# Attention and two feed-forward layers on one core: unread products among the lead's small steps, and window loads four slots later

## The chip, the cores and the metric

One core of one Trainium2 chip. The time is device microseconds of that core, for one launch that computes everything. The core has TensorE (matrix products into PSUM), VectorE, ScalarE and GpSimd, and SyncE (SP), whose queue issues all of this kernel's DMAs in program order.

## What is computed

Inputs q, k, v are 4 batches x 8 heads x 576 positions x 64, in f32.

```python
q_d, k_d, v_d = (a.reshape(B, H, Sd, 4, D).mean(axis=3) for a in (q, k, v))
out_up = np.repeat(sm_attn(q_d, k_d, v_d), 4, axis=2)      # coarse attention
mask = np.abs(pos[:, None] - pos[None, :]) < 4             # local attention
out_local = softmax(where(mask, scale * q @ k.T, -1e9)) @ v
x = (out_up + out_local) as (B, S, 512)
x = x + relu(layernorm(x) * g_ln @ w_ch1) @ w_ch2          # first layer, 512 -> 2048 -> 512
x_prev = x shifted by one position
k2 = relu((mu_k * x + (1 - mu_k) * x_prev) @ w_k)          # second layer, 512 -> 1024 -> 512
out = sigmoid((mu_r * x + (1 - mu_r) * x_prev) @ w_r) * ((k2 * k2) @ w_v)
```

## The kernel before

The 2304 rows are worked on in eight units u of 288 rows (half a batch each); a unit has three windows of 96 rows, 24 windows in all. In the layers each f32 operand is split into a high and a low part, and every product is three fast ones (`prods`, L1062): high by high, high by low, low by high.

**The lead.** Unit 0's attention comes first, written out by hand on each engine. On TensorE (from L1160) it is: transposes of k and q (`turn`), local scores (`scores`), coarse scores (`scores_d`), transposes of the probabilities (`turn_p` for local, `turn_d` for coarse ones), the added values of half the heads (`add_values`), the value products (`values`, `values_d`), and at the end three products with ones that sum x over its features (`mean_first`). Between them the other engines mask, exponentiate, sum and copy. `FIRST` (L66) lists these steps with the pair of PSUM banks each uses: 0 is psA, 1 is psH, 2 and 3 are the halves of psY. The small steps use the first bank of their pair, except where `[:, 1]` or both are named; `added_bank` is the second bank of pair 2 until ScalarE has copied it (`added_o`, which signals `vd_first`). `masked` counts VectorE's masked scores.

**The first layer** has 128 steps m (unit u = m // 16, f = m % 16): `up_b(m)` makes 128 hidden features in psH by 12 products, `down_b(m - 1)` adds the features before to psY by 12 more. Between these two halves `attend(slot)` does small pieces of the next unit's attention: slot 2m and 2m + 1, 32 slots for a unit. `LATER` (L74) lists the slot of each piece: for unit u, relative to slot 32(u - 1), scores at 5 and 11, turns at 13 and 19, coarse values at 15, value products AV(u,0) at 15 and AV(u,1) at 21 (windows 1 and 2 of the unit together), the mean at 24. Unit 1's pieces come two slots later (`BEHIND`). `variance(0)` of unit 0 comes in slot 2, behind `up_b(1)`; it needs the sum of squares `sq_sum(0)` that GpSimd makes.

**What feeds the pieces.** All in the order of the slots too:

- `load_later(j)` (L588): a raw quarter of q or k in eight DMAs into one of three buffers `raw`. It waits until VectorE has transposed (`flip`, L1486) the piece three places before. `FLIPS` gives the slots, relative to slot 32u, so before the slot in which the layer takes up unit u: k at -18, -16, -14, -12 for even units alone, q at -10 and -7 for all; `FLIPS_THIRD` is unit 2's, k at -12, -10, -8, -4 and q at -3, -1. So k pieces for units 2, 4, 6 are loaded in the slots in which units 1, 3, 5 are attended.
- `load_v_sum(b, g)` (L600): values for the coarse attention, one DMA into `v_raw`, once GpSimd has summed (`v_sum`) the one before. `V_LOAD` and `V_SUM` give the slots.
- `load_window(w)` (L608): the local values of window w in four DMAs into `v_win`, which has two buffers from window 3 on. It waits for the value product that last read the buffer (`av_done`), so AV(u,0) is followed by the load of window 3u + 2, which AV(u,1) reads, and AV(u,1) by those of windows 3u + 3 and 3u + 4. `values` waits for each window that it reads (`wait_vw`).

SP's program (from L688) goes through the slots and issues in each, in this order, the raw pieces, the sums' values, the windows, and the small loads and stores of the layer. It waits in program order, so what stands behind a wait waits too.

**The second layer** follows with tiles of 512 rows; the change doesn't touch it.

Of the kernel before, what the change touches and what calls it, by code (L numbers as in the profile page):

```python
# [21 lines left out]
def fused_kernel(nc, q, k, v, g_ln, w_ch1, w_ch2, mu_k, mu_r, w_k, w_v, w_r, od_scr, x2_scr, out):  # L22
# [14 lines left out]
    NW_U = 3  # L37
# [52 lines left out]
    ROOT_OUT, ROOT_IN = 3, 10  # L90
    BEHIND = 2

    TURN = {"Tk": [(0, 1), (2, 3), (4, 5)], "Tq": [(0,), (1, 2)]}

    later = []
# [32 lines left out]
    def flips_at(slot):  # L128
        return [x[1:] for x in flips_by_slot if x[0] == slot]
# [8 lines left out]
    def steps_at(slot):  # L138
        return [x[1:] for x in later if x[0] == slot]
# [25 lines left out]
    V_SUM, V_LOAD = {}, {}  # L165
    for b in range(1, B):
        behind = BEHIND if b == 1 else 0
        for g, (s, load) in enumerate(((16 + behind, 8), (22 + behind, 17 + behind), (28 + behind, 21 + 2 * behind), (39, 31))):
            V_SUM[SLOTS * (2 * b - 2) + s] = (b, g)
            V_LOAD[SLOTS * (2 * b - 2) + load] = (b, g)  # L170

# [19 lines left out]
    with ExitStack() as ctx:  # L191
        def sem(name):
            return ctx.enter_context(nc.semaphore(name))

        def sb(scope, name, shape, dt=F32):
            return scope.enter_context(nc.sbuf_tensor(name, shape, dt))
# [60 lines left out]
        kT = sb(ctx, "kT", [P, KT, S])  # L257
# [9 lines left out]
        ident = sb(ctx, "ident", [P, P])  # L267
# [20 lines left out]
        pairs = [psA[:], psH[:], psY[:, 0:2], psY[:, 2:4]]  # L288
# [33 lines left out]
        vd_first = sem("vd_first")  # L322
# [12 lines left out]
        masked = sem("masked")  # L335
# [157 lines left out]
        def turn_source(what, n, x):  # L493
            return (k_first if what == "Tk" else q_first)[0:W, TURN[what][n][x]]

# [85 lines left out]
        def _(sp):  # L581
            def load_first(what, n, x):
                t0 = TURN[what][n][x] * W
                src = (k if what == "Tk" else q)[0, :, t0:t0 + W, :]
# [103 lines left out]
            for slot in range(-LEAD, SLOTS * NU):  # L688
                for x_ in flips_at(slot):
                    if HALF <= flip_of[x_] < len(flips) - RAW:  # L690
                        load_later(flip_of[x_] + RAW)
                if slot in V_LOAD:
                    load_v_sum(*V_LOAD[slot])
                for kind, u, n in steps_at(slot):
                    for part in parts_of(kind, u, n):
                        if kind == "AV" and NW_U * u + part + 2 < NWIN:
                            load_window(NW_U * u + part + 2)
                for kind, u, _ in steps_at(slot - ROOT_OUT):
                    if kind == "V":
                        store_rstd(u)  # L700
                if slot >= SLOTS and slot % SLOTS == 1:
                    store_x2(slot // SLOTS - 1)
                for kind, u, _ in steps_at(slot - ROOT_IN):
                    if kind == "V":
                        load_rstd(u)
                if slot == SLOTS * (NU - 1) + 2:
                    sp.wait_ge(av_done, count_by("AV", NU))
                    sp.wait_ge(x_made, NWIN)
                    sp.wait_ge(lead_zero, 1)
                    load_shifted(0)  # L710
                    load_shifted(1)
                f = slot - SLOTS * (NU - 1)
                if f in (8, 16):
                    j = f // 8 - 1
                    sp.wait_ge(h_ready, M_LAST + 4 * (j + 1))
                    sp.dma_start(wk_raw[:, :, j * 512:(j + 1) * 512],
                                 w_k[:, j * 512:(j + 1) * 512].rearrange("(a p) f -> p a f", p=P)).then_inc(wk_in[j], 16)
                    sp.wait_ge(h_used, M_LAST + 4 * (j + 1))
                    sp.dma_start(wv_raw[:, 4 * j:4 * j + 4],
                                 w_v[512 * j:512 * (j + 1), :].rearrange("(a p) e -> p a e", p=P)).then_inc(wv_in[j], 16)  # L720
                if f == 24:
                    sp.wait_ge(h_ready, M_LAST + 12)
                    sp.dma_start(wr_raw[:, :, :], w_r.rearrange("(a p) f -> p a f", p=P)).then_inc(wr_in, 16)
            store_x2(NU - 1)

            for c in range(NC):
                g0, n = tiles[c]
# [160 lines left out]
        def _(pe):  # L888
            mm = nc.tensor.matmul

            def turn(what, n):
                i = place_of[what, 0, n]
                pe.wait_ge(first_in[turn_of[what, 0, n]], 16 * len(TURN[what][n]))
                wait_bank_out(pe, i)
                for x in range(len(TURN[what][n])):
                    src = turn_source(what, n, x)
# [21 lines left out]
            def turn_d(u, n):  # L918
                i = place_of["PdT", u, n]
                pe.wait_ge(d_normed, 2 * u + n + 1)  # L920
                wait_bank_out(pe, i)
                p = coarse(prob_slot("Sd", u, n), u, n)
                for par in range(2):
                    for j in range(2):
                        for kh in range(2):
                            at = (2 * j + kh) * GU
                            ins = nc.tensor.transpose(pairs[pair_at(i)][0:GU, par, at:at + GU], p[:, par, j, kh * GU:(kh + 1) * GU],  # L927
                                                      ident[0:GU, 0:GU])
                ins.then_inc(pdt_done, 1)

            def add_values():
                for half in range(2):
# [49 lines left out]
            def turn_p(u, n):  # L982
                i = place_of["PT", u, n]
                w = NW_U * u + n
                pe.wait_ge(normed, w + 1)
                wait_bank_out(pe, i)
                p = prob_slot("S", u, n)[0:ROWS]
                for j in range(KT):
                    ins = nc.tensor.transpose(turned_bank(i)[:, j * ROWS:(j + 1) * ROWS],  # L989
                                              p[:, 2 * j * RB:2 * j * RB + RB + KB], ident[0:ROWS, 0:ROWS])  # L990
                ins.then_inc(pt_done, 1)

            def values(u, n):
                i = place_of["AV", u, n]
                for part in parts_of("AV", u, n):
                    pe.wait_ge(pt_out, NW_U * u + part + 1)
                    wait_vw(pe, NW_U * u + part)
                wait_bank_out(pe, i)
                for part in parts_of("AV", u, n):
                    vw = vw_slot(NW_U * u + part)  # L1000
                    pt = turned_place("PT", u, part)
                    place = local_place("AV", u, part, BQ)
                    for j in range(KT):
                        for par in range(2):
                            for bl in range(BLOCKS):
                                row = RB * (par ^ bl)
                                keys = slice(row, row + KB)
                                at = j * ROWS + bl * RB
                                ins = mm(place[D * par:D * par + D, bl, j], vw[keys, bl, j, :], pt[keys, at:at + BQ],  # L1009
                                         start=True, stop=True, skip_group_check=True)  # L1010
                ins.then_inc(av_done, 1)
# [5 lines left out]
            def mean_first(n):  # L1017
                i = place_of["M", 0, n]
                if n + 1 < NW_U:
                    pe.wait_ge(x_summed, n + 1)  # L1020
                else:
                    pe.wait_ge(last_summed, 1)
                wait_bank_out(pe, i)
                mm(pairs[pair_at(i)][:, 0, 0:W], ones[:], xs[:, 0, n * W:(n + 1) * W], start=True, stop=True).then_inc(mean_done, 1)
# [146 lines left out]
            turn_p(0, 0)  # L1171
            add_values()
            turn_d(0, 0)
            turn_d(0, 1)
            values(0, 0)
            turn_p(0, 1)
            values_d(0, 0)
            values_d(0, 1)
            turn_p(0, 2)
            values(0, 1)  # L1180
            values(0, 2)
            pe.wait_ge(consts, 7)
            mean_first(0)
            mean_first(1)
            mean_first(2)
            for slot in range(-LEAD, 0):
                attend(slot)
            for m in range(M_ALL):
# [21 lines left out]
        def _(act):  # L1210
            copy = nc.scalar.copy

            def turn_o(what, n):
                i = place_of[what, 0, n]
                act.wait_ge(turned, turn_of[what, 0, n] + 1)
                c0, nx = TURN[what][n][0], len(TURN[what][n])
                src = pairs[pair_at(i)][:, 0:nx, 0:KT * W].rearrange("p x (j y) -> p x j y", y=W)
# [251 lines left out]
        def _(dve):  # L1469
# [11 lines left out]
            def sum_first(what, n):  # L1481
                dve.wait_ge(turn_out, turn_of[what, 0, n] + 1)
                src, dst = (kT, kdT) if what == "Tk" else (qT, qdT)
                group_sum(src, dst, TURN[what][n][0] * GW, len(TURN[what][n]) * GW)

# [342 lines left out]
```

## Time and profile before

| | us |
|---|---|
| median of 3 runs (lowest to highest) | 768.27 (767.16 to 768.62) |
| the profiled execution | 768.22 |
| its span, first to last instruction | 766.0 |
| TensorE busy | 751.8 |
| VectorE, ScalarE, GpSimd busy | 431.0, 272.6, 232.3 |

The profile is one execution. A group of instructions is named by its line, its engine (PE is TensorE, DVE VectorE, ACT ScalarE, POOL GpSimd, SPq SP's queue) and out<-in by the kernel's names. Matrix products are pipelined: their records overlap, and a product's own duration is longer than the distance to the next. The granted clock of TensorE is given as a share of 2.4 GHz.

### The profile page before, as it was taken

To read this page: it belongs to the slowest core of one execution; us is meant where nothing else is said; L and a number is where in the kernel's file an instruction comes from. 1 tells how busy PE (TensorE), PEld (TensorE's weight loads), DVE (VectorE), ACT (ScalarE), POOL (GpSimd) and SP (SyncE) were. 2 spreads that over 40 slices of the span, in tenths; PEclk is the share of its full clock that TensorE was granted. 3 is DMA by queue.
4 is the path that set the end of the run, shared out by engine and by line. 5 is a ranking of instruction groups with operands and counts; after the bars stand their busy time and mean duration, and the time that the engine had idled before them with its cause. 6 is when DMAs were issued, how large, how long until landed. Compare 5 with 4: busy or idle time off the path is not lost.

```text
span 766.0 us, 15806 instructions
## 1 busy us (share of the span) xinstructions
PE 751.8 (98%) x6433; PEld 693.8 (91%) x6433; DVE 431.0 (56%) x805; ACT 272.6 (36%) x620; POOL 232.3 (30%) x268
## 2 busy tenths in 40 slices
PE   7799999999999999999999999999999999999998
PEld 6699999999999999999999999998888888888886
DVE  5676764444654354554354332567686676766655
ACT  3665423223233223233233231546334434333322
POOL 5666753132444223345223222004111111111101
PEclk9699999999999999999999999999999999999999
DMA  9992451220440121341011003612003011010010
GB/s 188 236 288 59 80 116 18 47 60 11 89 109 20 29 41 55 65 99 40 14 26 39 15 2 138 231 56 87 0 1 110 0 52 33 0 56 1 0 56 28
DMA packets 116543, 49.67 MB, mean 65 GB/s; under 512 B 95084, under 2 KB 105592, under 8 KB 116472
## 3 DMA queue, kind: packets, MB, share of 16 engines
q1 hardware_dynamic: 116472, 48.68, 24.8%
q8 instruction: 51, 0.84, 0.5%
q14 instruction: 20, 0.16, 0.1%
HBM read 39.20 MB, written 9.45 MB: 64 GB/s over the span
## 4 chain that ended last, share of the span: by engine, by line
PE 93%; SPq 2%; DVE 2%; DMA 1%; POOL 1%; issue 1%; ACT 0%; DVEq 0%; ACTq 0%
PE psH L1081 26%; PE psY L1098 25%; PE psH L1132 13%; PE psY L1153 13%; PE psA L1114 6%; PE psA L978 2%; PE psA L1009 2%; PE psA L954 1%; PE psA L914 1%; SPq L597 1%; PE psA L989 1%; PE psA L927 1%; DMA k_first<-in_k_dram 1%; SPq L585 1%; DMA v_raw<-in_v_dram 1%
## 5 line engine op out<-in xcount | busy, mean ns | idle before, releaser
L1081 PE MATMUL psH<-xc_hi,w_hi 128*128 128x288 f32 x512 | 156.0, 305 | 2.6 <-DVE xc_lo L1596 2.6
L1098 PE MATMUL psY<-h_hi,w_hi 128*128 128x288 f32 x512 | 153.2, 299 | 0.3 <-DVE y_tmp L1643 0.2
L1081 PE MATMUL psH<-xc_lo,w_hi 128*128 128x288 f32 x512 | 152.0, 297 | 0.0
L1081 PE MATMUL psH<-xc_hi,w_lo 128*128 128x288 f32 x512 | 151.9, 297 | 0.0
L1098 PE MATMUL psY<-h_lo,w_hi 128*128 128x288 f32 x512 | 150.8, 294 | 0.0
L1098 PE MATMUL psY<-h_hi,w_lo 128*128 128x288 f32 x512 | 150.7, 294 | 0.0
L1741 DVE SCALAR_TENSOR_TENSOR h_lo<-psH,h_hi 128x288 fp32r<-128x288 f32 x128 | 58.3, 456 | 164.0 <-ACT h_hi L1437 163.6
L1437 ACT ACTIVATE h_hi<-psH 128x288 fp32r<-128x288 f32 x128 | 52.5, 410 | 247.1 <-PE psH L1081 246.4
L883 POOL TENSOR_TENSOR relu_k<-relu_k 128x512 f32<-128x512 f32 (+1 forms) x39 | 38.6, 990 | 243.8 <-ACT relu_k L1392 243.8
L1081 PEld LDWEIGHTS psH<-xc_hi,w_hi 128*128 128x128 f32 x512 | 97.0, 190 | 5.3 <-issue 4.1
L1098 PEld LDWEIGHTS psY<-h_hi,w_hi 128*128 128x128 f32 x512 | 96.1, 188 | 2.5 <-issue 1.3
L1081 PEld LDWEIGHTS psH<-xc_lo,w_hi 128*128 128x128 f32 x512 | 97.2, 190 | 0.0
L1081 PEld LDWEIGHTS psH<-xc_hi,w_lo 128*128 128x128 f32 x512 | 97.2, 190 | 0.0
L1098 PEld LDWEIGHTS psY<-h_lo,w_hi 128*128 128x128 f32 x512 | 96.1, 188 | 0.1
L1098 PEld LDWEIGHTS psY<-h_hi,w_lo 128*128 128x128 f32 x512 | 96.1, 188 | 0.0
L1696 DVE RECIPROCAL gate<-gate 128x256 f32<-128x256 f32 x36 | 63.1, 1753 | 1.2
L1153 PE MATMUL psY<-w_hi,kh_hi 128*128 128x512 f32 x144 | 56.3, 391 | 0.2 <-DVE kh_lo L1772 0.2
L1153 PE MATMUL psY<-w_lo,kh_hi 128*128 128x512 f32 x144 | 56.1, 389 | 0.0
L1153 PE MATMUL psY<-w_hi,kh_lo 128*128 128x512 f32 x144 | 56.1, 389 | 0.0
L1392 ACT ACTIVATE relu_k<-psH 128x512 f32<-128x512 f32 (+2 forms) x41 | 22.3, 545 | 59.4 <-PE psH L1132 59.4
L1679 DVE SCALAR_TENSOR_TENSOR mixin<-x_sh,params,mixin 128x512 f32<-128x512 f32 (+1 forms) x40 | 34.8, 870 | 14.5 <-ACT mixin L1362 13.2
L824 POOL TENSOR_TENSOR x<-x,y_tmp 128x288 f32<-128x288 f32 x32 | 25.6, 830 | 45.6 <-DVE y_tmp L1643 45.6
(189 smaller groups left out, 1343.7 us busy)
## 6 DMA issues: line engine op xcount, KB each, us to landing
w_raw<-in_moe_w_ch_dram SPq DMA_DIRECT2D x8, 1024.0 KB, 8.7
v_win<-in_v_dram SPq DMA_DIRECT2D x84, 56.0 KB
x_scratch<-x SPq DMA_DIRECT2D x8, 576.0 KB, 4.2
out_dram<-gate SPq DMA_DIRECT2D x17, 256.0 KB, 2.2
raw<-in_q_dram SPq DMA_DIRECT2D x112, 36.0 KB, 2.0
raw<-in_k_dram SPq DMA_DIRECT2D x96, 36.0 KB, 1.9
v_raw<-in_v_dram SPq DMA_DIRECT2D x12, 288.0 KB
x_sh<-x_scratch SPq DMA_DIRECT2D x3, 1026.0 KB, 5.6
```

Of the source, the lines that this page charges most:

```text
L824: nc.gpsimd.tensor_tensor(x[:, u % 2, d], x[:, u % 2, d], y_tmp[:, d % 2], ALU.add).then_inc(x2_made, 1)
L883: nc.gpsimd.tensor_tensor(r, r, r, ALU.mult).then_inc(k_square, 1)
L1081: ins = mm(psH[:, m % 2, 0:N], ws[a][:, kt, f * P:(f + 1) * P], xx[bb][:, kt], start=(kt == 0 and i == 0), stop=(kt == KT - 1 and i == 2))
L1098: ins = mm(psY[:, d, 0:N], ws[a][:, f, d * P:(d + 1) * P], hs[bb][:, m % 2], start=(f == 0 and i == 0), stop=(f == NF1 - 1 and i == 2))
L1114: ins = mm(psA[:, u % 2, :], xx[a][:, kt, t * P:(t + 1) * P], ws[bb][:, kt, :], start=(kt == 0 and i == 0), stop=(kt == KT - 1 and i == 2))
L1132: ins = mm(psH[:, m % 2, 0:n], ws[a][:, kt, f * P:(f + 1) * P], xx[bb][:, kt, 0:n], start=(kt == 0 and i == 0), stop=(kt == KT - 1 and i = ...
L1153: ins = mm(psY[:, t, :], hs[a][:, m % 2, t * P:(t + 1) * P], ws[bb][:, f, :], start=(f == 0 and i == 0), stop=(f == NF2 - 1 and i == 2))
L1392: nc.scalar.activation(relu_k[:, m % 2, at], psH[:, m % 2, at], ACT.Relu).then_inc(k_relu, 1)
L1437: nc.scalar.activation(h_hi[:, m % 2], psH[:, m % 2, 0:N], ACT.Relu).then_inc(h_hi_ready, 1)
L1679: nc.vector.scalar_tensor_tensor(out=y, in0=x_sh[:, c % 2, kt, 1:n + 1], scalar=(muk_col, mur_col)[which][:, kt:kt + 1], in1=y, op0=ALU.mu ...
L1696: chain(nc.vector.reciprocal(g, g))
L1741: nc.vector.scalar_tensor_tensor(out=h_lo[:, m % 2], in0=psH[:, m % 2, 0:N], scalar=0.0, in1=h_hi[:, m % 2].bitcast(F32), op0=ALU.max, op1 ...
```

## The change

It adds a helper, `keep_on(n, pair)`, that issues n products of the identity with 256 columns of kT in f32 into the second bank of a pair; nothing reads the result. It is called in seven places of the lead, with 1, 1, 1, 1, 1, 1 and 5 products (11 in all), the first behind a wait for the third mask and the second behind one for `vd_first`. In SP's program the loads of windows are issued for the value products of the slot four before (`AV_LOAD`). For the second batch (b = 1), v_sum of g = 1 goes from slot 24 to 22 and the load of g = 2 from slot 25 to 23.

```diff
--- before.py
+++ after.py
@@ -89,6 +89,10 @@
 
     ROOT_OUT, ROOT_IN = 3, 10
     BEHIND = 2
+
+    AV_LOAD = 4
+
+    KEEP = 256
 
     TURN = {"Tk": [(0, 1), (2, 3), (4, 5)], "Tq": [(0,), (1, 2)]}
 
@@ -165,7 +169,7 @@
     V_SUM, V_LOAD = {}, {}
     for b in range(1, B):
         behind = BEHIND if b == 1 else 0
-        for g, (s, load) in enumerate(((16 + behind, 8), (22 + behind, 17 + behind), (28 + behind, 21 + 2 * behind), (39, 31))):
+        for g, (s, load) in enumerate(((16 + behind, 8), (22, 17 + behind), (28 + behind, 21 + behind), (39, 31))):
             V_SUM[SLOTS * (2 * b - 2) + s] = (b, g)
             V_LOAD[SLOTS * (2 * b - 2) + load] = (b, g)
 
@@ -691,7 +695,7 @@
                         load_later(flip_of[x_] + RAW)
                 if slot in V_LOAD:
                     load_v_sum(*V_LOAD[slot])
-                for kind, u, n in steps_at(slot):
+                for kind, u, n in steps_at(slot - AV_LOAD):
                     for part in parts_of(kind, u, n):
                         if kind == "AV" and NW_U * u + part + 2 < NWIN:
                             load_window(NW_U * u + part + 2)
@@ -928,6 +932,11 @@
                                                       ident[0:GU, 0:GU])
                 ins.then_inc(pdt_done, 1)
 
+            def keep_on(n, pair):
+
+                for _ in range(n):
+                    mm(pairs[pair][:, 1, 0:KEEP], ident[:], kT[:, 0, 0:KEEP], start=True, stop=True, skip_group_check=True)
+
             def add_values():
                 for half in range(2):
                     g = 2 * half + 1
@@ -1171,18 +1180,27 @@
             turn_p(0, 0)
             add_values()
             turn_d(0, 0)
+            pe.wait_ge(masked, NW_U)
+            keep_on(1, 3)
             turn_d(0, 1)
             values(0, 0)
+            pe.wait_ge(vd_first, 1)
+            keep_on(1, 2)
             turn_p(0, 1)
             values_d(0, 0)
             values_d(0, 1)
             turn_p(0, 2)
+            keep_on(1, 2)
             values(0, 1)
             values(0, 2)
             pe.wait_ge(consts, 7)
+            keep_on(1, 2)
             mean_first(0)
+            keep_on(1, 2)
             mean_first(1)
+            keep_on(1, 2)
             mean_first(2)
+            keep_on(5, 2)
             for slot in range(-LEAD, 0):
                 attend(slot)
             for m in range(M_ALL):
```

## Rows read from the trace of the kernel before

**Rows 1.** page: busy per engine; clock in tenths per slice; a costly group

```profile
PE 751.8 (98%) x6433; PEld 693.8 (91%) x6433; DVE 431.0 (56%) x805; ACT 272.6 (36%) x620; POOL 232.3 (30%) x268
...
PEclk9699999999999999999999999999999999999999
...
L1081 PE MATMUL psH<-xc_hi,w_hi 128*128 128x288 f32 x512 | 156.0, 305 | 2.6 <-DVE xc_lo L1596 2.6
```

**Rows 2.** TensorE's waits: us in total, times, longest

```profile
PE psH L1081 <- DVE xc_lo L1596: 2.6, 1, 2.6
```

**Rows 3.** half-microsecond windows: each engine's busy us, then granted clock, DMA share

```profile
23.50:24.00 0.50, 0.50 (x29) 0.50 (x32) 0.00 (x0) 0.46 (x1) 0.50 (x2) 0.72 0.31 57
40.50:41.00 0.50, 0.50 (x4) 0.50 (x4) 0.50 (x1) 0.50 (x2) 0.15 (x1) 0.71 1.04 345
```

**Rows 4.** timeline of TensorE in the lead: start us, us, what, [idle before]

```profile
22.81 0.70 PE L927 MATMUL psH<-ident,prob_first 72*72 72x72 f32 x8 [0.41 <-POOL prob_first L782]
...
24.28 1.00 PE L989 MATMUL psY<-ident,prob 112*120 112x112 f32 x4
...
29.21 1.07 PE L1009 MATMUL psH<-probT_first,vw_first 56*64 56x48 f32 x32
...
36.06 0.58 PE L1081 MATMUL psH<-xc_hi,w_hi 128*128 128x288 f32 x1 [2.56 <-DVE xc_lo L1596]
...
41.44 0.65 PE L1038 MATMUL psA<-xs,ones 128*128 128x288 f32 x2
```

**Rows 5.** chain that ended last, in order of time, in the first layer

```profile
47.71 1.59 PE psH L1081 x12
```

**Rows 6.** timeline of TensorE at full clock: small steps of later units

```profile
71.27 1.27 PE L954 MATMUL psA<-probT,vd 72*64 72x72 f32 x32
72.47 0.68 PE L1009 MATMUL psA<-y_tmp,v_win 56*64 56x48 f32 x32
...
126.14 0.55 PE L989 MATMUL psA<-ident,prob 112*120 112x112 f32 x4
```

**Rows 7.** timeline of VectorE: the last x of the lead

```profile
30.35 0.62 DVE L1568 TENSOR_TENSOR x<-psH,odT 128x192 f32<-128x192 f32 x2 [0.23 <-PE psH L1009]
```

**Rows 8.** timeline of GpSimd: the end of the sum of squares

```profile
39.84 0.80 POOL L813 TENSOR_TENSOR xs<-xs 128x288 f32<-128x288 f32 x1
```

**Rows 9.** timeline of SP's queue in the units u = 1, 3, 5

```profile
79.78 3.80 SPq L597 DMA_DIRECT2D raw<-in_k_dram  x8
...
195.16 1.82 SPq L616 DMA_DIRECT2D v_win<-in_v_dram  x4
197.03 4.11 SPq L597 DMA_DIRECT2D raw<-in_q_dram  x8
...
201.66 8.53 SPq L597 DMA_DIRECT2D raw<-in_q_dram  x16
...
318.30 3.90 SPq L597 DMA_DIRECT2D raw<-in_q_dram  x8
...
322.71 9.11 SPq L597 DMA_DIRECT2D raw<-in_q_dram  x16
```

**Rows 10.** page, DMA issues: KB each, median us from issue to landing

```profile
raw<-in_q_dram SPq DMA_DIRECT2D x112, 36.0 KB, 2.0
```

**Rows 11.** timeline of TensorE: value products AV(u,1) of u = 1, 3, 5

```profile
83.61 1.15 PE L1009 MATMUL psA<-probT,v_win 56*64 56x48 f32 x64
...
202.80 1.15 PE L1009 MATMUL psA<-probT,v_win 56*64 56x48 f32 x64
...
324.11 1.15 PE L1009 MATMUL psA<-probT,v_win 56*64 56x48 f32 x64
```

**Rows 12.** timeline of VectorE: the transposes that release SP's raw loads

```profile
194.97 0.77 DVE L1491 STREAM_TRANSPOSE kT<-raw 128x576 f32<-128x576 f32 x1
...
316.28 0.77 DVE L1491 STREAM_TRANSPOSE kT<-raw 128x576 f32<-128x576 f32 x1
```

**Rows 13.** timeline of GpSimd: a sum of local values

```profile
101.72 1.28 POOL L774 TENSOR_TENSOR v_raw<-v_raw 72x512 f32<-72x512 f32 x1 [3.60 <-DMA v_raw<-in_v_dram]
```

## The prediction, made before the changed kernel ran

> **What bounds the kernel now.** Read the page first: TensorE is busy in 98% of the span, and the clock line is at 9 tenths in every slice but one [rows 1]. Then TensorE's own waits: behind the first layer's start none is over 0.2 us, and the longest after the opening one is the 2.6 us ahead of the first layer, for the last low part of x [rows 2]. So nearly every microsecond that an engine or a queue adds to TensorE's path is a microsecond of the result, and the only slack that can be bought back lies in the lead. The windows of half a microsecond show what is off there: the granted clock falls to 0.50 (1.2 GHz) inside 23.5 to 24.0 us and is back at 1.00 (2.4 GHz) inside 40.5 to 41.0 us [rows 3]. Before the fall TensorE did small steps with gaps between them; before the rise it had run dense products from 36.06 us.
>
> The profiled execution took 768.22 us, its span 766.0 us; the median of the runs is 768.27 us. My sum starts at 768.2.
>
> **Part 1, products in the lead.** Eleven products that nobody reads, 256 columns in f32 each. The nearest row is the 288-column f32 product of two instructions at 41.44 us, 0.65 us from first start to last end [rows 4]. The layer's products last 0.305 us [rows 1] but start every 0.13 (1.59 for twelve [rows 5]), so some 0.17 of it overlaps what follows: 0.48, and for 256 columns 0.43 us at 2.4 GHz, 0.86 at 1.2 GHz (estimates). Both added waits stand one step ahead of a place where TensorE awaits the same thing anyhow (the masks before values(0,0), the copy of the added values before the second coarse value product), and none of its waits names either [rows 2], so I cost them at nothing; what would show it wrong is an idle time of TensorE behind VectorE's mask or ScalarE's copy. Of the eleven, one falls into the gap of 0.41 us ahead of the second small transpose at 22.81 us [rows 4], two lie in the dense run of small steps, three sit around the mean products and five between the last mean product and the first layer.
>
> If the clock stays at 2.4 GHz: from the turn at 24.28 to the end of the values at 30.28 us is 6.0 us at half clock [rows 4]. The same steps in later units cost 0.55 for a turn (two of them), 1.2 for both coarse value products, and about 0.61 each for two value products [rows 6]: 3.5 us. Two added products make it 4.4, a gain of 1.6. What follows is VectorE's work (its sums, centring and low parts run from 30.35 us [rows 7] to the first layer's start), so the first layer starts at 34.5 in place of 36.06; the three products around the means and the five after them (2.2 us, from about 31.5 to 33.7) fit in TensorE's idle time there. The first 24 products then cost twice 1.59 us [rows 5] and not 5.38 (36.06 to 41.44 us [rows 4]): 2.2 us less. But not all of it is kept. The variance product behind them needs the sum of squares that GpSimd ends at 40.64 us [rows 8], and that chain depends on GpSimd's and ScalarE's order, not on TensorE: it moves by 1.6 only, to 39.0, while TensorE would be there at 37.7. A new wait of 1.4 us takes part of the gain. Net: 41.44 to 39.04, **2.4 us gained**.
>
> If the clock still falls and stays down until the dense stretch, the two products on the path cost 1.7 us, the three around the means make the last mean late, and five at 0.86 run to about 39.9 us, 3.8 late, of which the products at full rate give back 2.2: 1.6 us lost. If it comes back just before the last five, 0.4 us are gained. Ends: 2.4 gained, 1.6 lost. I take 2.4, since the added products stand just where the activity was thin.
>
> The Trainium skill (TensorE: Matmul & The Clock Gate, Part 4) says that transposes do not count as busy for the clock. Here the stretch before the fall is half small transposes, which agrees; by that rule one added product there may be too little, and the lead would give 0.4 in place of 2.4, as in the third rival.
>
> **Part 2, the window loads four slots later.** A slot is half an m step, about 1.9 us. A value product AV(u,0) at slot 15 frees a buffer of v_win, and SP loads window 3u+2 into it, which AV(u,1) at slot 21 reads (17 and 23 in the first unit attended beside the layers). Before, that load was the next thing in SP's queue. Now it stands at slot 19 (21), behind what SP does in between. With no raw k loads due there (u = 2, 4, 6, 7) nothing is in between, and it costs nothing. For u = 1, 3, 5 there is, and each group of raw loads is eight issues and waits for VectorE's transpose.
>
> u = 1: in between stand one v_raw load and one group of raw loads, which ran from 79.78 for 3.80 us [rows 9], released by VectorE's transpose. So the window's four issues start at 83.62. They take 1.82 us [rows 9]; the last starts 1.4 after the first, and a load lands 2.0 us after its issue (the raw loads' median, the nearest row [rows 10]): 3.4 us in all, landing at 87.0. TensorE wants it at 83.61 [rows 11]. **Stall 3.4 us.**
>
> u = 3: two groups of raw loads and one v_raw. The transpose ends at 195.74 [rows 12]; a group of 4.11 us, then 0.5 for v_raw (the gap from 201.14 to 201.66), then half of the sixteen in 8.53 us [rows 9]: 195.78 + 4.11 + 0.5 + 4.27 = 204.66. Landed at 208.1, wanted at 202.80 [rows 11]. **Stall 5.3 us.**
>
> u = 5, the same way: 317.05 + 3.90 + 0.5 + 4.56 = 326.05, landed at 329.45, wanted at 324.11 [rows 9, 11, 12]. **Stall 5.3 us.** Together **14.0 us**, all exposed, since TensorE runs in order and behind the value product stand the layer's products; ScalarE, VectorE and GpSimd wait with it. Ends: 12.5 (landing in 1.7, groups in 3.8) to 16 (the four window issues in 2.5).
>
> The other four groups of window loads (windows 3u+3 and 3u+4, from slot 21 to 25) are wanted a unit later, some 40 us, and cost nothing. The raw loads behind them come earlier; only VectorE could use that, off the path.
>
> **Part 3, the clock after the stalls.** No row shows a fall in the middle of the layers, because TensorE never stops there. The bounds: nothing, or what the first layer paid, 2.2 us each (5.38 against 3.18 [rows 4, 5]). A stall of 5.3 us with no product at all is emptier than the stretch before 23.7 us, so I take 2.2 for each of the two long ones and nothing for the short one: **4.4 us**. Ends 0 and 6.6.
>
> **Part 4, local sums of the second batch.** v_sum(1,1) goes from slot 24 to 22 on GpSimd and the load of (1,2) from slot 25 to 23 on SP. GpSimd waited 3.60 us for such a load at 101.72 us [rows 13]; that wait shrinks, yet TensorE had none behind it [rows 2], so 0. What hides the earlier sum is GpSimd's idle time; without it the x sums behind would be late by the sum's two microseconds, which is half a step of a layer, and the mean product that reads them stands several slots later: still 0.
>
> **Sum.** 768.2 - 2.4 + 14.0 + 4.4 = 784.2 us.
>
> **Rivals.**
> 1. The other side: the windows land in time. SP has to reach the window's first issue 3.4 us before the value product, that is by 80.2, 199.4 and 320.7 us; then only the lead counts and the time is 765.8. For it: SP has idle time between its groups in the units that hold no raw k loads. Against it: in u = 1, 3, 5 the transposes' ends fix the groups' starts, and they are too late by 3 to 5 us. 5%.
> 2. Stalls as computed, clock held through them: 768.2 - 2.4 + 14.0 = 779.8. For it: the fall in the lead followed many small gaps, not one. 20%.
> 3. The products don't do what they are for: the clock falls at about 24 us all the same and comes back only before the layer; 768.2 - 0.4 + 14.0 + 4.4 = 786.2. For it: half of that stretch is transposes. 20%.
> 4. The clock falls at all three stalls and the lead loses: 768.2 + 1.6 + 14.0 + 6.6 = 790.4. 15%.
>
> My own case has 38%; 2% are left for no change that can be told, where stalls shrink to the lead's gain. About 0.2% is what a measurement of this kernel can tell from no change, 1.5 us. Faster by more than that is only the first rival, a little under its 5% since the lead may give less: 4%; within 0.2%: 2%; slower: 94%. The likeliest case's sum is the forecast, 784.2. The range reaches from the clock-held case with the low end of the stalls (768.2 - 2.4 + 12.5 = 778.3, rounded down for a shorter landing) to the worst case with the high end (768.2 + 1.6 + 16 + 6.6 = 792.4): 777 to 793.
>
> **What the changed profile would show.** TensorE's waits hold three for the DMA of v_win at its value products, 3 to 6 us each, near 81, 204 and 330 us, and none in the units between. In SP's queue those windows' issues stand behind the raw loads. The clock of the slices behind those stalls drops below 1.00 for a few microseconds. The clock of 24 to 36 us is 1.00, the first layer starts near 34.5 us and a wait for GpSimd's sum stands before the variance. I am wrong if those value products wait for nothing, or if the rest grows in a place that I did not name.

## The result, and the profile after

The changed kernel takes 787.87 us in the median of 4 runs (786.16 to 788.60), the kernel before 767.76; the ratio is 1.0258, with a 95% interval of 1.0237 to 1.0279. The profiled execution took 787.55 us with a span of 785.4, 19.4 us more than before. The forecast was 784.2, the range 777 to 793.

The page after, beside [rows 1]: TensorE is busy for 5 us more in a span 19 us longer, and the clock line has an 8 among its nines in slices 11 and 18, where before there was a 6 in slice 2.

```profile
span 785.4 us, 15850 instructions
...
PE 756.7 (96%) x6455; PEld 697.5 (89%) x6455; DVE 431.7 (55%) x805; ACT 272.2 (35%) x620; POOL 232.5 (30%) x268
...
PEclk9999999999899999989999999999999999999999
```

TensorE's own waits (us in total, times, longest), beside [rows 2]:

```profile
PE psA L1018 <- DMA v_win<-in_v_dram: 15.3, 3, 6.5
...
PE psA L918 <- DVE var_e L1641: 1.5, 1, 1.5
...
PE psH L1090 <- DVE w_lo L1648: 0.8, 1, 0.8
PE psH L1090 <- DVE xc_lo L1614: 0.5, 1, 0.5
```

The 2.6 us ahead of the first layer have become 0.5, but two waits for VectorE are new, and above all stand three waits for `v_win`. In TensorE's timeline they are the value products AV(u,1) of u = 1, 3, 5, and no others [rows 11]:

```profile
86.28 1.15 PE L1018 MATMUL psA<-probT,v_win 56*64 56x48 f32 x64 [3.85 <-DMA v_win<-in_v_dram]
...
212.81 1.96 PE L1018 MATMUL psA<-probT,v_win 56*64 56x48 f32 x64 [6.53 <-DMA v_win<-in_v_dram]
...
340.97 1.96 PE L1018 MATMUL psA<-probT,v_win 56*64 56x48 f32 x64 [4.90 <-DMA v_win<-in_v_dram]
```

SP's queue shows why, for u = 3 [rows 9]:

```profile
199.18 5.02 SPq L601 DMA_DIRECT2D raw<-in_q_dram  x8
204.56 0.31 SPq L609 DMA_DIRECT2D v_raw<-in_v_dram  x1
204.92 3.93 SPq L601 DMA_DIRECT2D raw<-in_q_dram  x8
208.89 1.82 SPq L620 DMA_DIRECT2D v_win<-in_v_dram  x4
```

Two groups of raw loads and a v_raw load stand ahead of the window. It is issued from 208.89 us and is there for 212.81; TensorE had asked at 206.28. The second and third products also last 1.96 us in place of 1.15, which is the clock. One-microsecond windows (the column after the busy times is the granted clock) show it at half behind the stalls, and when it comes back:

```profile
90.00:91.00 1.00, 1.00 (x7) 1.00 (x6) 0.02 (x1) 0.46 (x2) 0.26 (x1) 0.54 0.39 89
216.00:217.00 1.00, 1.00 (x6) 1.00 (x5) 0.00 (x0) 0.00 (x0) 0.92 (x3) 0.50 0.00 0
217.00:218.00 1.00, 1.00 (x8) 1.00 (x8) 0.00 (x0) 0.30 (x1) 0.92 (x3) 0.89 0.00 0
...
346.00:347.00 1.00, 1.00 (x6) 1.00 (x5) 0.41 (x2) 0.73 (x2) 0.99 (x1) 0.54 0.00 0
```

TensorE worked at 1.2 GHz from 87.5 to 90.9, 212.8 to 217.2 and 341.0 to 346.9 us, 13.7 us in all, and lost up to half of that, 6.9 us. In the two long waits the clock fell while TensorE still stood (at about 210.4 and 340.1 us), at the short one 1.2 us after the wait had ended.

The account, from the starts of the value products in the two traces: AV(1,0) comes 1.25 us earlier than before, then the stretches from AV(1,0) to AV(2,0), AV(3,0) to AV(4,0) and AV(5,0) to AV(6,0) are longer by 4.65, 8.50 and 7.58 us, and all others are equal. That is -1.25 + 20.73 = 19.5 us. Of the 20.7, the waits are 15.3. The second batch's slots take 0.8 off the first stretch (experiment 5), so 6.2 us are left for the clock: 1.6, 2.0 and 2.7, each a little under half of its stretch at 1.2 GHz (1.7, 2.2 and 2.95).

In the lead the clock stayed at 1.00 in this execution:

```profile
33.66 0.38 PE L1090 MATMUL psH<-xc_hi,w_hi 128*128 128x288 f32 x1 [0.53 <-DVE xc_lo L1614]
...
35.92 0.40 PE L1090 MATMUL psH<-xc_hi,w_hi 128*128 128x288 f32 x1 [0.83 <-DVE w_lo L1648]
...
38.20 0.72 PE L1047 MATMUL psA<-xs,ones 128*128 128x288 f32 x2
...
43.93 0.71 PE L918 MATMUL psA<-kdT,qdT 64*72 64x144 f32 x8 [1.49 <-DVE var_e L1641]
```

The layer begins at 33.66 us and not 36.06 [rows 4], and the variance product at 38.20 and not 41.44, 3.2 us earlier. But the next small piece, unit 1's first coarse scores, starts at 43.93; before it was 45.19. Of 3.2 us, 1.3 are left. VectorE and GpSimd in that stretch (two timelines, VectorE's first):

```profile
34.10 1.77 DVE L1648 SCALAR_TENSOR_TENSOR w_lo<-w_raw,params,w_hi 128x512 fp32r<-128x512 f32 x1
```

```profile
33.72 1.61 POOL L834 TENSOR_TENSOR w_lo<-w_raw,w_hi 128x512 fp32r<-128x512 f32 x1 [1.09 <-ACT w_hi L1349]
```

VectorE's low part of w1 lasted 1.77 us beside GpSimd's low part of w2; others of the same shape take 0.74. The two low parts from 38.87 us took 1.81 and 1.77, beside GpSimd's next two.

### The profile page after: what moved, and what is told of

It reads as the page before. It is cut to its first block, busy times and chain, and to the rows that moved or that the text cites. A ratio compares the mean times of both kernels' runs of the same rounds, so it can differ in the third digit from the quotient of the medians.

```text
span 785.4 us, 15850 instructions
## 1 busy us (share of the span) xinstructions
PE 756.7 (96%) x6455; PEld 697.5 (89%) x6455; DVE 431.7 (55%) x805; ACT 272.2 (35%) x620; POOL 232.5 (30%) x268
## 4 chain that ended last, share of the span: by engine, by line
PE 90%; SPq 4%; DVE 3%; DMA 1%; issue 1%; POOL 1%; ACT 0%; DVEq 0%; ACTq 0%
PE psH L1090 26%; PE psY L1107 24%; PE psH L1141 13%; PE psY L1162 12%; PE psA L1123 6%; SPq L601 2%; PE psA L1018 2%; PE psA L987 2%; PE psA L963 1%; PE psA L918 1%; PE psA L931 1%; DMA v_win<-in_v_dram 1%; PE psA L998 1%; DVE w_lo L1648 1%; DMA k_first<-in_k_dram 1%
```

## The experiments

Twelve kernels in three groups (1 to 4; 6 to 9; 5 and 10 to 12). The kernel before was run beside each group, 85 times in all: its medians are 767.82, 767.69 and 767.14 us, and each ratio is taken against its own group. Milestones in a trace (the start of AV(1,0), of the first coarse scores) take the lead's own variation out of a comparison, which the totals can't.

**1. The loads back at their place** (`e1`):

```diff
-    AV_LOAD = 4
+    AV_LOAD = 0
```

> The changed kernel with the window loads at their old place in SP's queue (AV_LOAD = 0); lead products and the second batch's slots stay. Theory (the three stalls and what the clock loses behind them are the whole slowing, 20.7 us between the units in the two traces; the lead gives 1.25): about 1.25 us below the kernel before, 766.5 us, ratio near 0.998, no wait of TensorE for v_win. Rival (the products or the second batch's slots cost something as well, hidden in the sum): 769 us or more.

Measured: 767.21 us, ratio 0.9996 (0.9984 to 1.0008), no wait for v_win. The theory of the slowing holds: without the late windows nothing of the 20 us is left. The gain of 1.25 us is not there in the median, though. Its eleven runs reach from 766.24 to 770.28, and the profiled one was the longest, which shows what varies. The clock in its lead:

```profile
21.00:22.00 1.00, 0.84 (x9) 0.84 (x10) 0.96 (x3) 1.00 (x4) 1.00 (x2) 0.87 0.95 213
22.00:23.00 1.00, 1.00 (x6) 0.62 (x6) 0.27 (x2) 0.57 (x2) 1.00 (x2) 0.50 0.80 168
31.00:32.00 1.00, 1.00 (x48) 1.00 (x46) 0.23 (x1) 0.99 (x2) 0.04 (x1) 0.51 1.06 410
32.00:33.00 1.00, 1.00 (x28) 0.89 (x21) 0.97 (x4) 0.87 (x2) 0.53 (x1) 1.00 1.18 290
```

The lead's instructions are the same as in the changed kernel, and still the clock fell at 21.7 us and was back at 32.0. The products on the path went at 1.2 GHz, and the first coarse scores started at 47.87 us, 3.9 later than in the changed kernel's trace and 2.7 later than before. So the products hold the clock in some executions, and cost where they don't. The mean clock that is recorded with every run says in how many: in six of the eleven it is 0.999 or 1.0, and these took 766.24 to 767.21 us; in the other five it is 0.993 to 0.997, and they took 767.62 to 770.28. Of the 85 runs of the kernel before none is above 0.996. Against the kernel before's 767.82, the median of the six is 1.4 us less, that of the five 1.2 us more.

**2. The late loads alone** (`e2`): the kernel before, with only

```diff
-                for kind, u, n in steps_at(slot):
+                for kind, u, n in steps_at(slot - 4):
```

> The kernel before with the window loads alone four slots later. Theory: the stalls need nothing of the lead, so 768 + 20.7 = 788.5 to 789.5 us, three waits for v_win of 4 to 6.5 us, in u = 1, 3, 5. Rival (the earlier lead or the second batch's slots bring the queue and TensorE out of step): well under 788 and shorter waits, or none at u = 1.

Measured: 787.97 us, ratio 1.0258 (1.0235 to 1.0280), half a microsecond under the expected and the same as the whole change. The three waits:

```profile
87.68 1.96 PE L1009 MATMUL psA<-probT,v_win 56*64 56x48 f32 x64 [3.71 <-DMA v_win<-in_v_dram]
...
213.82 1.96 PE L1009 MATMUL psA<-probT,v_win 56*64 56x48 f32 x64 [5.27 <-DMA v_win<-in_v_dram]
...
341.75 1.96 PE L1009 MATMUL psA<-probT,v_win 56*64 56x48 f32 x64 [5.05 <-DMA v_win<-in_v_dram]
```

They make 14.0 us, and the clock fell at each. The late loads are the slowing, with or without the other parts. That the whole change takes no less than this kernel also says that its lead and slots bring nothing that its totals show: in the changed kernel's trace the gains of 1.25 and 0.8 us stand beside waits that are 1.3 us longer than here.

**3. The stalls filled with products** (`e3`):

```diff
+                wait_bank_out(pe, i)
+                if n == 1:
+                    for _ in range({1: 28, 3: 48, 5: 36}.get(u, 0)):
+                        mm(psA[:, 1, 0:N], w1_hi[:, 0, 0:P], xc_hi[:, (u - 1) % 2, 0], start=True, stop=True, skip_group_check=True)
+                for part in parts_of("AV", u, n):
                     wait_vw(pe, NW_U * u + part)
-                wait_bank_out(pe, i)
```

> The changed kernel, with unread dense products of 0.13 us issued on TensorE just ahead of the wait for v_win at AV(u,1): 28, 48 and 36 of them in u = 1, 3, 5 (3.7, 6.4, 4.8 us, a little less than the three stalls of 3.85, 6.53, 4.90). They take only time in which TensorE would stand. Theory (of the 20.7 us, 15.3 are the wait and 5.4 the half clock behind it): the clock stays at 1.00 through units 1, 3, 5, and the time falls by about 5.4 to 782.5 us, while the windows land as late as before. Rival (the 5.4 us come from something else than the clock, as late pieces of the other engines): the same 787.9 us or more.

Measured: 782.86 us (1.0180 to 1.0208 of before), 5.0 us under the changed kernel. The clock line of the page is 9 in every slice, and the mean clock of all four runs is 0.999 or 1.0 (0.987 to 0.989 in the changed kernel's four). At u = 3 the product follows its fillers with no wait (the view begins with the second of the 48), at u = 1 it waits for another 0.41 us, at u = 5 for 0.59:

```profile
204.75 6.43 PE L1009 MATMUL psA<-xc_hi,w_hi 128*128 128x288 f32 x47
211.11 1.15 PE L1022 MATMUL psA<-probT,v_win 56*64 56x48 f32 x64
```

The stalls' time is spent all the same, and the half clock is gone. That part is therefore the clock's: 5.0 by the medians, 5.7 by the two profiled executions, against 6.2 in the account above. The fillers and waits ahead of the three products took 4.30, 6.49 and 5.55 us, 16.3 in all and not 15.3; whether the 48 ran past the landing of their window the trace doesn't say. Between AV(1,0) and AV(7,0) e3's trace is 5.45 us shorter than the changed kernel's; with that 1 us set aside it is 6.5, and the account and the experiment agree within 0.3 us.

**4. Two slots instead of four** (`e4`): `AV_LOAD = 2`.

> The changed kernel with the window loads two slots later and not four (AV_LOAD = 2). Then in u = 1 only the v_raw load is ahead of them, in u = 3 and 5 one group of raw loads and a v_raw load, not two groups. Theory (what counts is which raw groups stand ahead in the queue): no wait in u = 1; in u = 3 and 5 the windows are issued about 4 us earlier, so the waits shrink from 6.5 and 4.9 to 1 to 2.5 us each, 769 to 772 us with whatever the clock does. Rival (each slot of delay costs in proportion): half of the slowing, about 777 us.

Measured: 774.86 us, ratio 1.0098 (1.0078 to 1.0118); no wait in u = 1, waits of 3.31 and 2.20 us in u = 3 and 5. SP's queue in u = 3:

```profile
194.37 5.11 SPq L601 DMA_DIRECT2D raw<-in_q_dram  x8
199.84 0.31 SPq L609 DMA_DIRECT2D v_raw<-in_v_dram  x1
200.21 1.78 SPq L620 DMA_DIRECT2D v_win<-in_v_dram  x4
```

One raw group ahead in place of two. TensorE asked at 201.46 us, so the window's first issue came 1.25 us ahead of that, where in the changed kernel's trace it came 2.6 behind: 3.9 us earlier. The expected order holds (nothing at u = 1, shorter waits at 3 and 5), the size was missed by 3 us: the window's four loads needed 4.6 us from first issue to use, not 3.4, and the clock fell behind the wait of 3.31 us (0.50 from 206 to 209 us), but not behind the one of 2.20. What fits is neither my 769 to 772 nor the proportional 777, but the waits as they are: in the profiled execution, 773.93 us, the stretches of units 3 and 5 are longer than a stretch without a stall by 4.89 and 2.26 us, which is 5.5 for the waits and 1.6 for the clock.

**5. The second batch's slots alone** (`e5`):

```diff
-((16 + behind, 8), (22 + behind, 17 + behind), (28 + behind, 21 + 2 * behind), (39, 31))
+((16 + behind, 8), (22, 17 + behind), (28 + behind, 21 + behind), (39, 31))
```

> The kernel before with the second batch's slots alone (v_sum(1,1) at 22, the load of (1,2) at 23). From the traces so far: with them GpSimd no longer waits 3.6 us for the load at 98 us, its sums into x start earlier, and TensorE's stretch from AV(1,1) to AV(2,0) is 46.6 us in place of 47.4. Theory (this part is worth 0.8 us, which the prediction costed at nothing): 766.9 us, ratio 0.999. Rival (the 0.8 us came with the shifted lead): no change.

Measured: 766.97 us, ratio 0.9996 (0.9987 to 1.0004): by the totals not to be told from no change, as both medians lie within 0.2 us. By the traces the part is there: from AV(1,0) to AV(7,0) it is 360.93 us, before it was 361.78. GpSimd's timeline:

```profile
96.41 1.30 POOL L774 TENSOR_TENSOR v_raw<-v_raw 72x512 f32<-72x512 f32 x1
...
101.25 3.08 POOL L824 TENSOR_TENSOR x<-x,y_tmp 128x288 f32<-128x288 f32 x4 [2.63 <-DVE y_tmp L1643]
```

The sum no longer waits 3.60 us for its load [rows 13]. Before, GpSimd came out of it at 103.8 us, late for its additions into x; VectorE's scaled values waited for those, and TensorE's first products of the next unit for VectorE. The stretch from AV(1,0) to AV(2,0) is 57.73 us in place of 58.54. In the nine other kernels that have these slots and no stall in unit 1 it is 57.7 to 58.1, so the slots are worth 0.5 to 0.8 us by ten traces against one; the totals neither confirm nor exclude it.

**6 and 7. Parts of the lead** (`e6` keeps only the five products ahead of the layer, `e7` only the six single ones; loads at their old place).

```diff
 # e6: the six calls keep_on(1, ...) and their two waits go
 # e7
-            keep_on(5, 2)
```

> e1 (window loads at their old place) without the six single products between the small steps; only the five ahead of the first layer stay. Theory (the clock falls at 22 to 24 us for want of the single products, and the five alone bring it back a little before the layer at best): half clock from about 23.7 to between 37 and 41 us; the five cost 0.86 each at half clock and end after 36.06, so the first layer starts later by 1 to 2 us and gains up to 2.2 back: 767.5 to 769 us, about the kernel before. Rival (the five do the work): as e1 at its best, 766.3 us.

> e1 without the five products ahead of the first layer; the six single ones stay. Theory (the six hold the clock in most runs, and between the last mean and the layer TensorE then stands for about 2.5 us, near the gap in which it may fall): 766.3 us in the runs in which it holds, 768 to 769 us where it falls in that gap and the layer's first products go at half clock; median 767 us. Rival (the five are needed in every run): 768.3 us throughout.

Measured: `e6` 767.14 us, 0.9988 (0.9978 to 0.9998); `e7` 767.01 us, 0.9989 (0.9977 to 1.0001). Both are nearer to the kernel before than the 0.2% that the prediction counts as the least to be told, and so is e1 with all eleven, 0.9996. In e6's trace the clock was at half from 23.2 to 36.9 us, as expected; in e7's it stayed at 1.00 up to 35.4 us and fell a microsecond behind the gap of 2.7 us ahead of the layer. Their first coarse scores start at 45.14 and 44.97 us, where the kernel before has 45.19. By the mean clocks no run of the two, 24 in all, is above 0.998, where e1 has six of eleven: neither group holds the clock up to the layer alone, and both together do so in part of the runs. e6 came out below its expected range of 767.5 to 769 us, e7's median where it was expected, with runs from 764.78 to 769.46.

**8. Low parts apart** (`e8`, on e1):

```diff
+            sq_sum(0)
             lo_w2(0)
-            sq_sum(0)
...
-    W1_M = {0: [(1, 0), (1, 1)], 1: [(1, 2)], 2: [(1, 3)], 3: ...
+    W1_M = {0: [(1, 0)], 1: [(1, 1)], 2: [(1, 2), (1, 3)], 3: ...
```

> e1 with GpSimd's sum of squares ahead of its first low part of w2, and with VectorE's low parts of w1 spread as one, one and two over the steps 0, 1 and 2 (two, one, one before). In the changed kernel VectorE's low part of w1 at 34.10 us took 1.77 us beside GpSimd's of w2, where it takes 0.74 alone, and so did the two at 38.9 and 40.6; TensorE waited 0.8 and 1.5 us behind them. Theory (that collision takes back half of the lead's gain): those two waits shrink to under 1 us together, and the time falls by 1 to 1.5 us against e1, to 765.0 to 765.5 us in the runs in which the clock holds. Rival (other waits of the same size take their place: the low part of w2 for down_b, later now): no change against e1.

Measured: 766.24 us, 0.9984 (0.9968 to 0.9999), runs from 764.18 to 769.39; the profiled one took 764.41. VectorE and, in the second fence, TensorE:

```profile
33.42 1.40 DVE L1648 SCALAR_TENSOR_TENSOR w_lo<-w_raw,params,w_hi 128x512 fp32r<-128x512 f32 x2
```

```profile
33.65 0.37 PE L1090 MATMUL psH<-xc_hi,w_hi 128*128 128x288 f32 x1 [0.53 <-DVE xc_lo L1614]
...
38.86 0.40 PE L1107 MATMUL psY<-h_hi,w_hi 128*128 128x288 f32 x1 [0.80 <-DVE h_lo L1759]
...
42.23 0.71 PE L918 MATMUL psA<-kdT,qdT 64*72 64x144 f32 x8
```

Two low parts take 1.40 us together where one took 1.77, the waits of 0.8 and 1.5 us are gone, one of 0.8 for h_lo is new, and the coarse scores start at 42.23 us, 1.7 earlier than in the changed kernel at the same clock. The two engines are not wholly apart: VectorE's next low part, at 38.73 us, ran beside GpSimd's and took 1.48. The Trainium skill (SBUF — State Buffer, Who interferes with whom) says that a VectorE instruction with two inputs in SBUF contends with a GpSimd instruction that reads SBUF; the traces agree, 1.77 us beside GpSimd's low part against 0.70 without it. The six runs in which the clock held took 764.18 to 765.81 us, beside e1's 766.24 to 767.21, and the expectation for them was met; the other six took 766.66 to 769.39, so the median moved little and the spread is 5.2 us in place of 4.0.

**9. The gap filled** (`e9`, on e1): two more products ahead of the first small transpose, the wait for the masks moved up with them.

```diff
+            pe.wait_ge(masked, NW_U)
+            keep_on(2, 3)
             turn_d(0, 0)
-            pe.wait_ge(masked, NW_U)
             keep_on(1, 3)
```

> e1 with two more unread products, between the added values and the first small transpose, where TensorE stands for 0.9 us (20.8 to 21.7 us) waiting for GpSimd. Theory (in some runs of e1, 769 to 770.3 us, as in its profile, the clock falls at 21.7 us since that gap and the transposes are thin; the two products fill it, 0.43 us each): the slow runs go, all within 766.0 to 767.0 us, and the clock is 1.00 from 20 to 40 us. Rival (what decides is the place of the chip's look and not this gap): still a spread up to 770 us.

Measured: 766.27 us, 0.9986 (0.9976 to 0.9997), nine of eleven runs from 765.91 to 767.24, two at 768.06 and 768.37. The runs of 769 to 770 us are gone, and the spread is 2.5 us in place of 4.0, not closed. By the mean clock eight of eleven runs held it, beside six of eleven in e1 and, with the same repair, seven and five of twelve in experiments 10 and 11. That the gap is part of the cause is possible, and not shown. In the profiled execution the clock is 1.00 from 19 to 49 us.

**10. Both repairs** (`e10`: e8 and e9 together).

> e1 with both repairs: the two more products in the gap before the first small transpose (e9) and the low parts apart (e8). Theory (e9 makes the clock hold in nearly all runs, e8 takes 1.8 us off those in which it holds): median 764.3 to 764.8 us, few runs over 766. Rival (the two don't add, since e8's repair opens the next wait, 0.8 us for h_lo): 765.5 us.

Measured: 764.79 us, ratio 0.9981 (0.9966 to 0.9996): the fastest kernel of the study, 23 us under the changed one and 0.2% under the one before, with an interval that ends just below 1. Seven of twelve runs are at 763.84 to 765.05, five at 766.45 to 768.68: the median is as expected, but five runs over 766 are not few. In the profiled one, of the slower kind, TensorE stood ahead of products into psY, and the clock fell inside that stop, at 39.2 us:

```profile
39.64 0.61 PE L1107 MATMUL psY<-h_hi,w_hi 128*128 128x288 f32 x1 [2.03 <-DVE h_lo L1760]
```

**11. The loads wanted a unit later, four slots later** (`e11`, on e10): only those behind AV(u,1).

> e10 with the window loads behind AV(u,1) alone four slots later (they are wanted a unit later); those behind AV(u,0) at their old place. Theory (only the loads wanted two slots later hurt; the others have 40 us and cost or give nothing): the same as e10, no wait for v_win. Rival (raw loads that come earlier help VectorE and with it TensorE): below e10 by half a microsecond or more.

Measured: 767.51 us, 0.9995 (0.9979 to 1.0011), no wait for v_win. The median is 2.7 above e10's, which was not expected. The traces put none of it on the loads: from AV(1,0) to AV(7,0) it is 360.94 us here and 361.02 in e10. All of the difference between the two profiled executions lies ahead of AV(1,0), where SP's program and the lead are the same in both. Both kernels have runs of two kinds, five of twelve near 764.5 us here and seven there, and the median falls into the larger group. In e11 VectorE waited there for raw q:

```profile
38.37 0.78 DVE L1510 STREAM_TRANSPOSE qT<-raw 128x576 f32<-128x576 f32 x1 [2.98 <-DMA raw<-in_q_dram]
```

behind it h_lo, and with it TensorE, which stood for 3.3 us and then worked at half clock up to 46.8 us. In e10's trace the same wait is 1.32 us, in e8's 0.35. So by the traces the late windows of this kind are harmless, as expected; and in these three traces, once the lead is short, the landing of raw q is what varies next. Why it varies was not tried.

**12. No products** (`e12`): e1 without any of the eleven, with the low parts apart.

> e1 without any of the eleven unread products, but with the low parts apart and the second batch's slots. Theory (without the products the clock falls and stays at half until about 40 us as before; the collision doesn't show then): 766.9 us, as e5. Rival (keeping the low parts apart helps by itself, and the products add little): 765.5 us.

Measured: 767.03 us, 0.9994 (0.9983 to 1.0004), runs from 764.76 to 768.07. In its trace the clock was 1.00 up to 32.2 us with no product added, then at half to 39 us. With e5's trace (1.00 to 31.4 us, back at 38.2, coarse scores at 43.77) this is the second execution without products in which the small steps alone held the clock through the means. Between e12 and e8, which differ in the products and their two waits alone, lie 0.8 us of median, inside both spreads. What the products do is plainer in the mean clock of the runs than in their medians:

| kernel | products | runs at 0.999 or 1.0 | their times, us | the other runs, us |
|---|---|---|---|---|
| before | 0 | 0 of 85 | | 764.84 to 770.25 |
| e5 | 0 | 0 of 11 | | 765.80 to 767.32 |
| e12 | 0 | 0 of 11 | | 764.76 to 768.07 |
| e6 | 5 | 0 of 12 | | 764.70 to 767.58 |
| e7 | 6 | 0 of 12 | | 764.78 to 769.46 |
| e1 | 11 | 6 of 11 | 766.24 to 767.21 | 767.62 to 770.28 |
| e9 | 13 | 8 of 11 | 765.91 to 766.69 | 767.24 to 768.37 |
| e8 | 11 | 6 of 12 | 764.18 to 765.81 | 766.66 to 769.39 |
| e10 | 13 | 7 of 12 | 763.84 to 765.05 | 766.45 to 768.68 |
| e11 | 13 | 5 of 12 | 764.10 to 764.99 | 767.47 to 769.36 |

Only with all of them does the clock hold from end to end, as far as the recorded clock tells, in 32 of 58 runs and in none of 131 without. A held clock is not all that decides the time, though: the fastest run of the kernel before, 764.84 us, is under every run of e1.

## Why the prediction was right, and where its terms were off

**The stalls** were the step that decided, and it stood: three, at the value products of u = 1, 3, 5, 15.3 us against 14.0. Singly 3.85, 6.53 and 4.90 against 3.4, 5.3 and 5.3. The term that was short is the landing: I took 3.4 us from the first window issue to landing, measured 3.9, 3.9 and 3.8 in the changed kernel and 4.6 in e4. At u = 3 a raw group also took 5.02 us and not 4.11. The total is nearer than the single stalls, since the one at u = 5 was forecast too long.

**The clock behind the stalls** was forecast for the two long ones at 2.2 us each, 4.4. It fell at all three, and filling them with products brought back 5.0 to 5.7 us. The mechanism was right; the short stall was judged wrongly (1.6 us and not 0), and the long ones cost 2.0 and 2.7 us for 4.4 and 5.9 us of work at half.

**The lead** was forecast at 2.4 us gained, with a new wait of 1.4 ahead of the variance. The trace gave 1.25, in an execution in which the clock held. The layer did start early (33.66, forecast 34.5), and the variance at 38.20 (39.0). What failed is the sentence that the sum of squares would be the next limit. It ended at 38.04 us, and no wait for it is listed before the variance product; the next limits were VectorE's low parts, stretched by GpSimd's, for which the sum has no term. At the same place in the trace of before the two had met for 0.7 us alone, and there it was GpSimd's that lasted longer (1.85 us), while VectorE's two took 1.41 together:

```profile
35.83 1.41 DVE L1630 SCALAR_TENSOR_TENSOR w_lo<-w_raw,params,w_hi 128x512 fp32r<-128x512 f32 x2
...
36.53 1.85 POOL L830 TENSOR_TENSOR w_lo<-w_raw,w_hi 128x512 fp32r<-128x512 f32 x1 [2.70 <-ACT w_hi L1331]
```

And I took what the clock did in one execution for a property of the kernel. Rival 3, that the clock falls all the same, is true of e1's profiled execution, though it came back before the last five products. Over the runs of e1 both cases of the prediction are there: 1.4 us gained in the median where the clock held, 1.2 lost where it didn't, and 0.6 gained over all, less than a measurement tells. That the fall comes from the transposes in that stretch, as the prediction reads the trace of before, is not borne out: e5 and e12 went through the same transposes, with no product added, at 1.00 up to 31.4 and 32.2 us.

**The second batch's slots** were costed at nothing because no single wait of TensorE was listed behind GpSimd's. They were there, in pieces: in the six microseconds from 102 us TensorE was busy for 5.53 before, and in e5 for all of the six from 99.5. The traces give 0.5 to 0.8 us.

**The sum**: 784.2 against 787.6 for the profiled execution; the stalls measured 1.3 more than forecast, the clock 1.8 more and the lead's gain 1.1 less, and the slots took 0.8 off that the sum doesn't have, together 3.4. That the last hides part of the first three is luck.

Rival 2 (779.8, the clock held through the stalls) was shown wrong by the windows of the clock and by e3. Rival 1 (windows in time) is wrong for four slots. Rival 4 (790.4) has the fall at all three stalls right and the lead's loss wrong for the profiled execution.

## What to carry to other kernels

A DMA that is moved later in an in-order queue is not later by its slots but by all that is now ahead of it: count the issues (eight of them took 3.8 to 5.0 us here) and the waits of what it passes, and compare with when its reader asks. Of two loads moved by one constant, the one wanted 11 us later and the one wanted 50 us later are different cases; only the first cost anything. Where one engine is busy in 98% of the span, a wait can also cost what the clock does behind it, here another 40% on top. And a change in the lead should be judged over many runs, by their mean clocks and by milestones in the trace, since one execution shows one course of the clock.

## What was not expected of the hardware

Executions with the same lead differ in where the clock falls, and with it by up to 4 us of the total: at 21.7 us and back at 32.0 in e1, not at all in the changed kernel; and, without any product, from 23.7 to 40.8 us in the kernel before but from 31.4 to 38.2 in e5.

Stops of an otherwise dense TensorE of 2.7 us (e7), 3.31 (e4) and 3.85 us (the changed kernel) were each followed by half clock, for 3.4 us of work in the last case. The length of the stop alone doesn't decide: the clock fell inside a stop of 2.03 us in e10, and didn't fall at all at this one of 2.20 in e4, where it reads 1.00 from 326 to 336 us:

```profile
329.87 1.15 PE L1018 MATMUL psA<-probT,v_win 56*64 56x48 f32 x64 [2.20 <-DMA v_win<-in_v_dram]
```

What sets the moment was not tried.

The granted clock of the views says nothing of the first microseconds. In the trace of before it reads 1.00 from 5 to 19 us, but the local scores took 1.97 us at 13.28, and the same 64 products take 1.15 in unit 1, at 63.22:

```profile
13.28 1.97 PE L978 MATMUL psY<-kT,qT 64*64 64x56 f32 x64
```

So the rows bear out 1.00 ahead of the fall at 23.7 us only from about 17 us on, where the next steps take their time at full clock.
